# A reordered three-layer kernel: input splits moved to GpSimd, transposes and a layer norm spread between matmuls, and a new memory map

## The chip, the cores and the metric

The kernel runs on one core of one Trainium2 chip. The metric is the device time of one execution in microseconds (us). TensorE (PE) multiplies, VectorE (DVE), ScalarE (ACT) and GpSimd (POOL) work on tiles, and SyncE (SP) issues the loads. DVE and ACT read the accumulation banks that PE fills; POOL works on tiles in the on-chip memory only. Pairs below are numbered q0 to q27 over the whole kernel.

## The reference

Three layers, cut to what matters here (b = 2 batches, 768 positions, 512 features, all float32):

```python
x  = window_and_block_attention(q, k, v)             # (2, 768, 512)
h  = relu(x.transpose(0, 2, 1) @ w_tok1) @ w_tok2    # mixing over positions
u  = x + h.transpose(0, 2, 1)
u  = u + relu(u @ w_ch1) @ w_ch2                     # 1536 hidden columns
xn = (u - mean(u)) / sqrt(var(u) + 1e-6) * g_ln
out = u + relu(xn @ w2_ch1) @ w2_ch2                 # 2048 hidden columns
```

## The kernel before, in words

Each float32 matmul is made of three matmuls of rounded parts: every operand is split into a high part (a cast, on ACT) and a low part (the value minus the high part, one subtraction with both inputs in on-chip memory). The functions with names `high_...` and `low_...` make these parts.

**The up products.** The two channel layers are four groups, g = 0 to 3: layer and batch (0 and 1 are layer one on batch 0 and 1; 2 and 3 are layer two). A group has 6, 6, 8 and 8 pairs of 128-column hidden blocks (`PAIRS_OF`). For one pair, `up(q, i)` multiplies seven combinations of weight blocks and input blocks (a two by two Strassen scheme), i = 0 to 6, six matmuls of 384 columns each. The seven inputs of a group, `in_t[:, i]`, are three raw blocks of the transposed input (`raw_in`) and four sums of them, `t_in`, which POOL makes in `sum_inputs`; `high_input` and `low_input` split each. The products land alternately in two banks (`up_bank`). ACT copies product 0 to `p1`; DVE adds the others to `u2`, `u3` and three `c_raw` tiles. ACT and DVE turn four blocks into `hidden` (relu, high and low).

**The down products.** While PE works at the ups of pair q, it does between them the twelve units `down(q-1, t, f)` of the pair before, three matmuls of 512 columns each, into six banks that hold the group's output. `DOWNS_AFTER` says how many follow each up. `low_down` (DVE) and `high_down` (ACT) split the down weights, `low_up`, `high_up`, `high_sums`, `low_sums` the up weights of the next pair. `sum_weights` and `low_sums` are POOL's, for every pair.

**The next group's input.** It is transposed on PE in eight batches of three 128x128 transposes (`turn_batch`), copied by ACT (`copy_batch`). `BATCHES_AT[g][j]` says how many stand at the end of pair j of group g. They use the same two banks as the ups. Before the groups of layer two the input is normalised: `norm_before` (DVE, six statistics, then the moments and the variance) stands at the end of the second pair of the next group, ACT takes a square root, and `norm_after` (DVE, `to_turn`) stands at the end of the third.

**Group ends.** In the first pair of a group, DVE adds the finished output tiles of the group before (`add_out`). The inputs 0 to 3 of the next group are split in the last pair of a group, 4 to 6 in its first (`LATE_IN`), all low parts on DVE.

**Before q0.** After the attention, PE multiplies the second batch's mixing (`mix_hidden`, 12 groups of three matmuls; `mix_out`, six tiles of six matmuls), with batches 0 to 7 of group 0's input between, and q0 follows.

Every engine runs its own list in order; semaphores join them. A wait on one engine holds all that stands behind it there. Two memory maps lie over each other: the tiles of the attention and the mixing, and the tiles of the channel layers. A tile of the second map may be written only when what lies under it in the first is no longer read.

Of the kernel before, what the change touches and what calls it, by code (L numbers as in the profile page):

```python
# [44 lines left out]
PAD = 640  # L45
# [37 lines left out]
def build(nc, q_t, k_w, v_w, v_edge, v_t, w_tok1, w_tok2, w_ch1, w_ch2, w2_ch1, w2_ch2, gain, mask,  # L83
          value_init, identity, out):
    ctx = ExitStack()
    with ctx:
# [19 lines left out]
        with ExitStack() as a:  # L106
# [15 lines left out]
            tok_stage = sb(a, "tok_stage", [P, S])  # L122
            tok_w = sb(a, "tok_w", [P, 2, TOK_CH, S], F32R)
            x_split = sb(a, "x_split", [P, B, 2, NT, DM], F32R)
# [78 lines left out]
        in_low = sem("in_low")  # L203
        up_done = sem("up_done")
# [56 lines left out]
        def _(sp):  # L261
# [99 lines left out]
        def _(pool):  # L361
# [62 lines left out]
            def sum_inputs(g):  # L424
                def blk(j, k):
                    return raw_in[:, 2 * j:2 * j + 2, k * HN:(k + 1) * HN]

                if g:
                    pool.wait_ge(in_low, 7 * g)
                tt = nc.gpsimd.tensor_tensor  # L430
# [5 lines left out]
                pool.wait_ge(t_made, 4 * g + 2)  # L436
                tt(t_in[:, 2], blk(1, 1), blk(0, 1), ALU.subtract).then_inc(t_made, 1)
                pool.wait_ge(t_made, 4 * g + 3)
                pool.wait_ge(in_copied, 8 * g + 8)
# [25 lines left out]
            sum_inputs(0)  # L465
            for q in range(1, NQ):
                g, j = group_of(q)
                if q + 1 < NQ:
                    sum_weights(q + 1)
                    low_sums(q + 1)  # L470
                if g + 1 < NGROUP and j == T_AT[g]:
                    sum_inputs(g + 1)


        @block.tensor
        def _(pe):
# [135 lines left out]
            for t in range(GT):  # L612
                mix_hidden(1, 1, t, score_bank[0])
            pe.wait_ge(x_low_end, 2)
# [3 lines left out]
            first_batch(2)  # L618
            first_batch(3)
            for t in range(NT):  # L620
                if t == 0:
                    pe.wait_ge(x_done, 2 * NPAIR)
                    pe.wait_ge(h_low, 4)
                if t >= 2:
                    pe.wait_ge(u_done, NT + t - 1)
                for m in range(2):
                    mix_out(t, m, o_bank[t % 2])
                if t < 4:
                    first_batch(4 + t)

            def up(q, i):
# [4 lines left out]
                if j == 0:  # L636
                    pe.wait_ge(in_low, 7 * g + i + 1)
# [23 lines left out]

            def pair(q):
# [3 lines left out]
                units = iter(UNITS)  # L666
                for i in range(7):
# [22 lines left out]
                    up(q, i)  # L690
                    if q:
                        for _ in range(DOWNS_AFTER[i]):
                            down(q - 1, *next(units))
                for b in range(BATCHES_AT[g][j]):
                    if g and turned % 8 == 0 and b == 0:
                        pe.wait_ge(nat_ready, NT * g)
# [4 lines left out]
                    turn_batch(turned + b)  # L701

# [7 lines left out]
        def _(act):  # L710
# [41 lines left out]
            def copy_batch(k):  # L752
# [3 lines left out]
                if g and i == 0:  # L756
                    act.wait_ge(in_low, 7 * g)
                    act.wait_ge(t_made, 4 * g)
# [39 lines left out]
            def pair(q):  # L798
# [12 lines left out]
                high_hidden(q, 0, product_bank(q, 2)[:, 0:HN])  # L811
                if q and q + 1 < NQ:
# [14 lines left out]
                if g in (1, 2) and j == 1:  # L827
                    act.wait_ge(ln_step, LN_STEPS * g)
                    nc.scalar.activation(dev[:], var[:], ACT.Sqrt).then_inc(dev_done, 1)
# [34 lines left out]
            copy_batch(1)  # L864
            for m in range(2):
                high_h(1, m, score_bank[1 - m])
                copy_batch(2 + m)
            high_input(0, 0)
            for k in range(4, 8):
                copy_batch(k)  # L870
            for i in range(1, 7):
# [6 lines left out]
        def _(dve):  # L878
# [85 lines left out]
            def norm_before(ln):  # L964

                dve.wait_ge(mixed, NT * (ln + 1))
                for j in range(NT):
                    nc.vector.bn_stats(stats[:, j, :], natural[:, NT * ln + j, :]).then_inc(ln_step, 1)
# [7 lines left out]
            def norm_after(ln):  # L976
# [15 lines left out]
                for j in range(NT):  # L992
                    nc.vector.tensor_scalar(to_turn[:, j, :], natural[:, NT * ln + j, :],  # L993
# [173 lines left out]
```

## Time and profile before

| | |
|---|---|
| median of 3 runs | 664.21 us (663.83 to 666.57) |
| profiled execution, its own time | 664.86 us |
| its span | 663.1 us |
| mean granted TensorE clock | 0.964 of full speed |
| PE busy | 598.0 us, 90% |
| DVE busy | 359.4 us, 54% |
| POOL busy | 247.2 us, 37% |
| ACT busy | 244.9 us, 37% |

The span lies within the execution's own time and is 1.76 us shorter. A busy figure is the sum of an engine's instructions; PE's is overstated a little, since the ends of its matmuls are modelled.

### The profile page before, as it was taken

Reading aid. Unit: us, or ns where it says so; the run is one execution under the profiler, and the core shown is the slowest. Engines: PE = TensorE matmul, PEld = TensorE weight load, DVE = VectorE, ACT = ScalarE, POOL = GpSimd, SP = SyncE. Lnnn points to the kernel's source line nnn. Section 1 sums busy time; section 2 is a strip of 40 time slices with the busy share of each in tenths; the row PEclk is TensorE's granted clock in tenths of the full one; section 3 lists DMA queues with packets and bytes.
Section 4 is the critical chain, followed back from the end, with each engine's and each line's share of the span. In section 5 each row is a group of like instructions: output and inputs, shape, how many; then the busy total and the mean of one; then the engine's idle time right before and its main releaser. Section 6 shows DMA issues by size and latency. Waiting matters only on the chain.

```text
span 663.1 us, 8253 instructions
## 1 busy us (share of the span) xinstructions
PE 598.0 (90%) x2976; PEld 513.7 (77%) x2976; DVE 359.4 (54%) x695; ACT 244.9 (37%) x450; POOL 247.2 (37%) x247
## 2 busy tenths in 40 slices
PE   5999998878999899986998798699998999999997
PEld 2777887757888787875787687588887788898896
DVE  5568656283444558654442876523445784444435
ACT  3577655242332235332323532233332633333321
POOL 5464744170333663320334533332227433333300
PEclk9899999898999989988999799889998999999999
DMA  8887540001111011111101111101111111111302
GB/s 230 238 232 217 162 130 2 1 0 64 63 65 63 2 63 64 64 63 64 63 20 46 64 63 64 63 1 64 64 64 63 65 63 65 64 64 63 128 0 96
DMA packets 24896, 50.34 MB, mean 76 GB/s; under 512 B 7596, under 2 KB 7832, under 8 KB 24856
## 3 DMA queue, kind: packets, MB, share of 16 engines
q1 hardware_dynamic: 24304, 49.37, 22.6%
q10 hardware_dynamic: 552, 0.44, 0.3%
q8 instruction: 24, 0.39, 0.2%
q14 instruction: 16, 0.13, 0.1%
HBM read 46.07 MB, written 3.15 MB: 74 GB/s over the span
## 4 chain that ended last, share of the span: by engine, by line
PE 65%; DVE 18%; ACT 8%; issue 5%; POOL 1%; DMA 1%; SPq 0%; DVEq 0%; ACTq 0%; POOLq 0%
PE bank L478 63%; DVE down_w L880 5%; DVE hidden L955 3%; ACT hidden L796 3%; DVE in_t L880 3%; ACT down_w L792 2%; DVE c_raw L1022 2%; DVE c_raw L1028 1%; PE bank L571 1%; DVE c_raw L1036 1%; DVE neg_scores L898 1%; DVE to_turn L993 1%; DMA k_sb<-k_w 1%; ACT probs L723 1%; PE bank L513 1%
## 5 line engine op out<-in xcount | busy, mean ns | idle before, releaser
L478 PE MATMUL bank<-down_w,hidden 128*128 128x512 f32 x1008 | 272.2, 403 | 3.4 <-DVE hidden L955 3.3
L478 PEld LDWEIGHTS bank<-down_w,hidden 128*128 128x128 f32 x1008 | 191.5, 193 | 34.5 <-issue 5.4
L478 PE MATMUL bank<-in_t,up_odd 128*128 128x384 f32 x588 | 124.5, 348 | 10.4 <-DVE c_raw L1022 4.3
L478 PE MATMUL bank<-in_t,up_even 128*128 128x384 f32 x588 | 122.1, 345 | 12.4 <-ACT p L802 5.5
L478 PEld LDWEIGHTS bank<-in_t,up_odd 128*128 128x128 f32 x588 | 108.8, 195 | 22.5 <-issue 9.6
L478 PEld LDWEIGHTS bank<-in_t,up_even 128*128 128x128 f32 x588 | 107.8, 194 | 23.1 <-ACT p L802 6.7
L796 ACT ACTIVATE hidden<-c_raw 128x384 fp32r<-128x384 f32 x84 | 44.2, 527 | 216.6 <-DVE c_raw L1022 118.2
L420 POOL TENSOR_TENSOR up_even<-sums_up,up_even 128x1024 fp32r<-128x1024 f32 x14 | 33.5, 2396 | 158.8 <-ACT up_even L786 158.7
L420 POOL TENSOR_TENSOR up_odd<-sums_up,up_odd 128x1024 fp32r<-128x1024 f32 x14 | 33.6, 2400 | 145.5 <-ACT up_odd L786 145.5
L955 DVE SCALAR_TENSOR_TENSOR hidden<-c_raw,hidden 128x384 fp32r<-128x384 f32 x84 | 59.0, 702 | 48.0 <-ACT hidden L796 48.0
L1003 DVE TENSOR_TENSOR u<-bank,p 128x384 f32<-128x384 f32 x28 | 15.6, 557 | 69.5 <-PE bank L478 68.0
L880 DVE TENSOR_TENSOR down_w<-raw_down,down_w 128x1024 fp32r<-128x1024 f32 x28 | 46.0, 1642 | 3.2 <-ACT down_w L792 2.6
L796 ACT ACTIVATE hidden<-bank 128x384 fp32r<-128x384 f32 x28 | 13.8, 492 | 86.0 <-PE bank L478 86.0
L478 PE MATMUL bank<-k_sb,q_sb 128*128 128x364 f32 x96 | 39.1, 493 | 5.7 <-POOL k_sb L369 3.1
L723 ACT ACTIVATE probs<-neg_scores,neg_max 128x182 f32<-128x182 f32 x96 | 37.8, 443 | 13.9 <-DVE neg_max L898 13.3
L898 DVE CUSTOM_DVE_ANT_0 neg_scores<-bank,mask_sb 128x182 f32<-128x182 f32 x96 | 29.3, 343 | 22.8 <-PE bank L478 20.9
L1022 DVE TENSOR_TENSOR c_raw<-bank,u 128x384 f32<-128x384 f32 x28 | 15.6, 556 | 42.1 <-PE bank L478 42.1
L1014 DVE TENSOR_TENSOR u<-bank,p 128x384 f32<-128x384 f32 x28 | 15.6, 557 | 37.2 <-PE bank L478 37.2
L955 DVE SCALAR_TENSOR_TENSOR hidden<-bank,hidden 128x384 fp32r<-128x384 f32 x28 | 15.6, 557 | 35.4 <-ACT hidden L796 35.4
L732 ACT COPY probs_t<-bank 128x384 f32<-128x384 f32 x48 | 22.8, 474 | 30.3 <-PE bank L513 30.1
L792 ACT CAST down_w<-raw_down 128x1024 fp32r<-128x1024 f32 x28 | 29.0, 1037 | 0.0
L478 PE MATMUL bank<-v_own,probs_t 128*128 128x65 f32 x192 | 27.5, 267 | 0.0
(87 smaller groups left out, 724.2 us busy)
## 6 DMA issues: line engine op xcount, KB each, us to landing
raw_up<-w_ch SPq DMA_DIRECT2D x28, 512.0 KB, 4.3
raw_down<-w_ch SPq DMA_DIRECT2D x28, 512.0 KB, 3.5
k_sb<-k_w SPq DMA_DIRECT2D x16, 273.0 KB, 4.3
v_own<-v_w SPq DMA_DIRECT2D x8, 390.0 KB, 3.3
q_sb<-q_t SPq DMA_DIRECT2D x8, 384.0 KB, 5.4
v_turned<-v_t SPq DMA_DIRECT2D x8, 384.0 KB, 3.4
out<-natural SPq DMA_DIRECT2D x12, 256.0 KB, 3.1
tok_stage<-w_tok SPq DMA_DIRECT2D x4, 384.0 KB, 3.9
```

Of the source, the lines that this page charges most:

```text
L420: nc.gpsimd.tensor_tensor(w[:, 1, 3:7, :], sums_up[:], w[:, 0, 3:7, :].bitcast(F32), ALU.subtract).then_inc(sums_low, 1)
L478: return nc.tensor.matmul(dst, lhs, rhs, start=start, stop=stop, skip_group_check=True)
L723: nc.scalar.activation(probs[:, n % 2, h * NK:(h + 1) * NK], neg_scores[:, n % 2, h, :], ACT.Exp, bias=neg_max[:, n % 2, h:h + 1], scale=- ...
L732: nc.scalar.copy(probs_t[:, n % 2, :], turn_bank[n % 2][:, 0:3 * P]).then_inc(turned_copied, 1)
L792: nc.scalar.copy(down_w[:, q % 2, :, 0, :], raw_down[:, q % 2]).then_inc(down_high, 1)
L796: nc.scalar.activation(hidden[:, q % 2, f, 0, h * HN:(h + 1) * HN], src, ACT.Relu).then_inc(hid_high, 1)
L880: return nc.vector.tensor_tensor(dst, src, high.bitcast(F32), ALU.subtract)
L898: nc.vector.tensor_tensor_reduce(neg_scores[:, n % 2, h, :], score_bank[n % 3][:, h * NK:(h + 1) * NK], mask_sb[:, kind, (1 - h) * NSUM:(1 ...
L955: nc.vector.scalar_tensor_tensor(out=hidden[:, q % 2, f, 1, at], in0=src, scalar=0.0, in1=hidden[:, q % 2, f, 0, at].bitcast(F32), op0=ALU ...
L1003: nc.vector.tensor_tensor(u2[:], product_bank(q, 1)[:, 0:HN], p1[:], ALU.add).then_inc(u_made, 1)
L1014: nc.vector.tensor_tensor(u3[:], product_bank(q, 3)[:, 0:HN], p1[:], ALU.add).then_inc(u_made, 1)
L1022: nc.vector.tensor_tensor(c_raw[:, 0], product_bank(q, 4)[:, 0:HN], u3[:], ALU.add).then_inc(c_made, 1)
```

## The change

The matmuls are the same in number and shape, and no load is added or left out. What changes is who does some steps, and where they stand:

- Of each group's seven low inputs DVE keeps 0 and 1 (`DVE_IN = 2`); POOL makes 2 to 6. They count on a semaphore of their own. In group 0, POOL makes 2 to 4 between its `t_in` sums.
- The six `mix_out` tiles of batch 1 stand after the ups 0 to 5 of q0. q0 has no transposes any more; group 0's pairs q1 to q4 have two batches each, group 1's q8 to q10 have 3, 3, 2.
- In pairs with batches the downs are spread: one or two stand behind each batch too.
- `norm_before` and `norm_after` are cut into pieces between the steps of the first two pairs of a group. The square root stands earlier on ACT.
- The second `c_raw` sum stands ahead of `low_down` on DVE.
- `sum_inputs` comes one pair earlier in groups 1 and 2.
- The memory map: `down_w` lies behind `raw_in`, under what the attention used; `hidden` lies higher, over parts of the second batch's x and the mixing weights; `x_split` and `tok_w` have changed places; `pad` is gone. The first two loads of `raw_down` wait for all four `mix_hidden` results (`tok1_done` 4) in place of the first two.

The core of the diff:

```diff
-DOWNS_AFTER = (2, 2, 2, 2, 1, 1, 2)
+DOWNS_AFTER = {0: (2, 2, 2, 2, 1, 1, 2), 2: (2, 2, 1, 1, 1, 1, 1, 1, 2), 3: (2, 1, 1, 1, 1, 1, 1, 1, 1, 2)}
-BATCHES_AT = ((2, 2, 2, 2, 0, 0), (0, 0, 2, 3, 3, 0), (0, 0, 2, 2, 2, 2, 0, 0), (0,) * 8)
-T_AT = (4, 5, 6)
+BATCHES_AT = ((0, 2, 2, 2, 2, 0), (0, 0, 3, 3, 2, 0), (0, 0, 2, 2, 2, 2, 0, 0), (0,) * 8)
+T_AT = (4, 4, 5)
+DVE_IN = 2
...
             raw_in = sb(b_, "raw_in", [P, C, S])
+            down_w = sb(b_, "down_w", [P, 2, 2, 2, DM], F32R)
+            in_t = sb(b_, "in_t", [P, 7, 2, 2, HN], F32R)
             t_in = sb(b_, "t_in", [P, 4, 2, HN])
-            in_t = sb(b_, "in_t", [P, 7, 2, 2, HN], F32R)
+            up_odd = sb(b_, "up_odd", [P, 2, 7, 2 * P], F32R)
+            raw_down = sb(b_, "raw_down", [P, 2, 2, DM])
             p1 = sb(b_, "p1", [P, HN])
             u2 = sb(b_, "u2", [P, HN])
             u3 = sb(b_, "u3", [P, HN])
+            c_raw = sb(b_, "c_raw", [P, 3, HN])
             hidden = sb(b_, "hidden", [P, 2, 2, 2, S], F32R)
-            pad = sb(b_, "pad", [P, PAD])
-            up_odd = sb(b_, "up_odd", [P, 2, 7, 2 * P], F32R)
-            raw_down = sb(b_, "raw_down", [P, 2, 2, DM])
-            down_w = sb(b_, "down_w", [P, 2, 2, 2, DM], F32R)
             to_turn = sb(b_, "to_turn", [P, NT, DM])
-            c_raw = sb(b_, "c_raw", [P, 3, HN])
...
                 else:
-                    sp.wait_ge(tok1_done, 2)
+                    sp.wait_ge(tok1_done, 4)
                 sp.dma_start(raw_down[:, q % 2], down_v[g // 2][j]).then_inc(ld_down[q % 2], 16)
...
+            def low_input(g, i):
+                pool.wait_ge(in_high, 7 * g + i + 1)
+                src = t_in[:, T_OF[i]] if i in T_OF else raw_block(i)
+                nc.gpsimd.tensor_tensor(in_t[:, i, 1], src, in_t[:, i, 0].bitcast(F32), ALU.subtract
+                                        ).then_inc(in_low_pool, 1)
+                pool.wait_ge(in_low_pool, (7 - DVE_IN) * g + i - DVE_IN + 1)
...
             sum_inputs(0)
+            low_input(0, 5)
+            low_input(0, 6)
             for q in range(1, NQ):
                 g, j = group_of(q)
+                if j == 0:
+                    for i in range(LATE_IN, 7):
+                        low_input(g, i)
                 if q + 1 < NQ:
                     sum_weights(q + 1)
                     low_sums(q + 1)
                 if g + 1 < NGROUP and j == T_AT[g]:
                     sum_inputs(g + 1)
+                if g + 1 < NGROUP and j == PAIRS_OF[g] - 1:
+                    for i in range(DVE_IN, LATE_IN):
+                        low_input(g + 1, i)
...
                     up(q, i)
+                    if q == 0 and i < NT:
+                        last_mix(i)
                     if q:
-                        for _ in range(DOWNS_AFTER[i]):
+                        for _ in range(after[i]):
                             down(q - 1, *next(units))
...
                     turn_batch(turned + b)
+                    for _ in range(after[7 + b]):
+                        down(q - 1, *next(units))
```

On ACT, the order ahead of q0 becomes copies 0 to 3, `high_input(0, 0)`, copy 4, `high_h(1, 0)`, copy 5, `high_input(0, 1)`, copy 6, `high_h(1, 1)`, copy 7, `high_input(0, 2)` to `(0, 6)`, and then the pairs. On DVE, a pair becomes, with the pieces for a group's second pair (`scaling`) shown:

```diff
                 nc.vector.tensor_tensor(u2[:], product_bank(q, 1)[:, 0:HN], p1[:], ALU.add).then_inc(u_made, 1)
-                if opening:
-                    for i in range(LATE_IN, 7):
-                        low_input(g, i)
+                if scaling:
+                    row_stats(g - 1, 4)
+                    row_stats(g - 1, 5)
...
+                if scaling:
+                    row_moments(g - 1)
                 dve.wait_ge(up_done, 7 * q + 4)
...
                 low_hidden(q, 1, c_raw[:, 0])
-                low_down(q)
...
                 dve.wait_ge(up_done, 7 * q + 6)
                 nc.vector.tensor_tensor(c_raw[:, 1], product_bank(q, 5)[:, 0:HN], u3[:], ALU.add).then_inc(c_made, 1)
-                if ending:
-                    low_input(g + 1, 2)
-                    low_input(g + 1, 3)
+                low_down(q)
                 low_hidden(q, 2, c_raw[:, 1])
...
-                if g in (1, 2) and j == 1:
-                    norm_before(g - 1)
-                if g in (1, 2) and j == 2:
-                    norm_after(g - 1)
```

`row_stats(ln, 0)` to `(ln, 3)` stand behind the `add_out` of the group's first pair, `row_scales` behind `u3` of the second, and two `normed` tiles behind each of its last three hidden blocks.

## Rows read from the trace of the kernel before

**Rows 1.** The page, busy time of the engine (share of the span) and instructions.

```profile
PE 598.0 (90%) x2976; PEld 513.7 (77%) x2976; DVE 359.4 (54%) x695; ACT 244.9 (37%) x450; POOL 247.2 (37%) x247
```

**Rows 2.** Windows: length, busy time by engine, granted clock (PEclk), DMA share, GB/s.

```profile
core 0: us, PE busy (x) PEld busy (x) DVE busy (x) ACT busy (x) POOL busy (x), PEclk, DMA share, GB/s
158.49:213.92 55.43, 51.92 (x253) 45.55 (x253) 23.10 (x34) 17.75 (x31) 16.68 (x15) 0.97 0.16 57
213.92:283.46 69.54, 65.61 (x312) 57.37 (x313) 43.00 (x55) 25.11 (x39) 31.94 (x24) 0.98 0.14 51
283.46:331.23 47.77, 38.79 (x173) 33.22 (x171) 24.07 (x49) 14.41 (x24) 10.90 (x10) 0.89 0.18 64
331.23:405.64 74.41, 67.89 (x321) 59.44 (x322) 41.72 (x54) 27.20 (x42) 32.76 (x24) 0.95 0.12 44
405.64:451.66 46.02, 36.99 (x169) 32.07 (x168) 24.07 (x49) 12.79 (x23) 10.89 (x10) 0.89 0.16 62
451.66:523.95 72.29, 67.23 (x325) 58.51 (x325) 35.30 (x44) 24.73 (x40) 31.95 (x24) 0.98 0.13 49
523.95:557.00 33.05, 31.96 (x156) 28.09 (x157) 22.54 (x34) 12.77 (x20) 12.16 (x10) 1.00 0.19 66
557.00:635.36 78.36, 78.36 (x392) 70.48 (x390) 37.83 (x56) 25.30 (x40) 24.63 (x21) 1.00 0.22 80
231.76:250.40 18.64, 17.74 (x79) 15.24 (x79) 11.34 (x14) 7.96 (x13) 11.06 (x10) 0.91 0.16 56
```

**Rows 3.** Timeline of q8, the layer norm: start, us, engine, line, [idle before <-releaser].

```profile
285.66 3.65 DVE L968 BATCH_NORM_STATS2 stats<-natural 128x6 f32<-128x512 f32 x6
...
290.59 1.60 PE L478 MATMUL bank<-in_t,up_even 128*128 128x384 f32 x6 [2.10 <-ACT p L802]
...
308.76 1.54 PE L571 MATMUL bank<-ident,to_turn 128*128 128x128 f32 x6 [5.56 <-DVE to_turn L993]
```

**Rows 4.** Timeline of PE: an up and two downs; the batches at the end of q1.

```profile
256.54 1.21 PE L478 MATMUL bank<-in_t,up_even 128*128 128x384 f32 x6
...
257.59 1.55 PE L478 MATMUL bank<-down_w,hidden 128*128 128x512 f32 x6
...
176.92 0.55 PE L571 MATMUL bank<-ident,natural 128*128 128x128 f32 x3 [0.69 <-DVE c_raw L1036]
...
177.94 1.28 PE L478 MATMUL bank<-in_t,up_even 128*128 128x384 f32 x6 [0.47 <-ACT raw_in L761]
```

**Rows 5.** Timeline of q4, where POOL makes the sums of the next input.

```profile
226.10 1.85 POOL L435 TENSOR_TENSOR t_in<-raw_in,t_in 128x768 f32<-128x768 f32 x1
226.13 2.24 DVE L955 SCALAR_TENSOR_TENSOR hidden<-c_raw,hidden 128x384 fp32r<-128x384 f32 x1 [0.59 <-ACT hidden L796]
...
228.03 2.04 POOL L437 TENSOR_TENSOR t_in<-raw_in 128x768 f32<-128x768 f32 x1
...
228.29 2.86 DVE L880 TENSOR_TENSOR down_w<-raw_down,down_w 128x1024 fp32r<-128x1024 f32 x1
...
231.76 1.29 PE L478 MATMUL bank<-in_t,up_odd 128*128 128x384 f32 x6 [1.95 <-DVE c_raw L1028]
```

**Rows 6.** Timeline of DVE, the same two operations with POOL idle.

```profile
300.46 1.23 DVE L880 TENSOR_TENSOR down_w<-raw_down,down_w 128x1024 fp32r<-128x1024 f32 x1 [0.39 <-ACT down_w L792]
...
304.37 0.56 DVE L955 SCALAR_TENSOR_TENSOR hidden<-c_raw,hidden 128x384 fp32r<-128x384 f32 x1 [0.59 <-ACT hidden L796]
```

**Rows 7.** Groups by line on POOL: count, busy us, mean ns of one, idle before.

```profile
L440 POOL TENSOR_TENSOR t_in<-raw_in,t_in 128x768 f32<-128x768 f32 x4 | 10.2, 2561 | 0.3
...
L435 POOL TENSOR_TENSOR t_in<-raw_in,t_in 128x768 f32<-128x768 f32 x4 | 7.4, 1843 | 3.1 <-ACT raw_in L761 2.8
```

**Rows 8.** Timeline ahead of q0 and in it.

```profile
121.22 6.37 PE L478 MATMUL bank<-x_split,tok_w 128*128 128x512 f32 x27
...
129.18 0.86 ACT L774 CAST in_t<-raw_in 128x768 fp32r<-128x768 f32 x1
...
142.55 0.47 ACT L802 COPY p<-bank 128x384 f32<-128x384 f32 x1
```

**Rows 9.** The page's loads: count, KB each, us from issue to landing.

```profile
raw_down<-w_ch SPq DMA_DIRECT2D x28, 512.0 KB, 3.5
```

More of the change, by code:

```diff
@@ L44 @@
 KB = 3
-PAD = 640
 AHEAD = 3
@@ L617, in _ @@
                     mix_hidden(1, m, t, score_bank[1 - m])
[L618 to L629, printed above, removed]
+                first_batch(4 + 2 * m)
+                first_batch(5 + 2 * m)
             def up(q, i):
@@ L635, in up @@
                 use[0] += 1
-                if j == 0:
-                    pe.wait_ge(in_low, 7 * g + i + 1)
+                if j == 0 and i < DVE_IN:
+                    pe.wait_ge(in_low, DVE_IN * g + i + 1)
+                if j == 0 and i >= DVE_IN:
+                    pe.wait_ge(in_low_pool, (7 - DVE_IN) * g + i - DVE_IN + 1)
                 for c in range(2):
@@ L660, in down, with last_mix @@
                     last.then_inc(down_done, 1)
+            def last_mix(t):
+                if t == 0:
+                    pe.wait_ge(x_done, 2 * NPAIR)
+                    pe.wait_ge(h_low, 4)
+                if t >= 2:
+                    pe.wait_ge(u_done, NT + t - 1)
+                for m in range(2):
+                    mix_out(t, m, o_bank[t % 2])
             def pair(q):
@@ L666, in pair @@
                 units = iter(UNITS)
+                after = DOWNS_AFTER[BATCHES_AT[g][j]]
                 for i in range(7):
@@ L690, in pair @@
                     up(q, i)
+                    if q == 0 and i < NT:
+                        last_mix(i)
                     if q:
-                        for _ in range(DOWNS_AFTER[i]):
+                        for _ in range(after[i]):
                             down(q - 1, *next(units))
                 for b in range(BATCHES_AT[g][j]):
-                    if g and turned % 8 == 0 and b == 0:
-                        pe.wait_ge(nat_ready, NT * g)
+                    if turned % 8 == 0 and b == 0:
+                        if g:
+                            pe.wait_ge(nat_ready, NT * g)
+                        else:
+                            pe.wait_ge(u_done, 2 * NT)
                     if b < 2:
@@ L811, in pair @@
                 high_hidden(q, 0, product_bank(q, 2)[:, 0:HN])
+                if g in (1, 2) and j == 1:
+                    act.wait_ge(ln_step, LN_STEPS * g)
+                    nc.scalar.activation(dev[:], var[:], ACT.Sqrt).then_inc(dev_done, 1)
                 if q and q + 1 < NQ:
@@ L863, in _ @@
             high_x(2 * NPAIR - 1)
-            copy_batch(1)
+            for k in range(1, 4):
+                copy_batch(k)
+            high_input(0, 0)
             for m in range(2):
+                copy_batch(4 + 2 * m)
                 high_h(1, m, score_bank[1 - m])
[L867 to L871, printed above, removed]
+                copy_batch(5 + 2 * m)
+                if m == 0:
+                    high_input(0, 1)
+            for i in range(2, 7):
                 high_input(0, i)
@@ L962, in add_out, with row_stats, row_moments @@
                 nc.vector.tensor_tensor(tile, acc_bank[t][:], tile, ALU.add).then_inc(mixed, 1)
[L964 to L968, printed above, removed]
+            def row_stats(ln, j):
+                dve.wait_ge(mixed, NT * ln + j + 1)
+                nc.vector.bn_stats(stats[:, j, :], natural[:, NT * ln + j, :]).then_inc(ln_step, 1)
+            def row_moments(ln):
                 for j in range(NT):
@@ L991, in norm_after, with normed @@
                     dve.wait_ge(in_turned, 8 * (ln + 2))
-                for j in range(NT):
-                    nc.vector.tensor_scalar(to_turn[:, j, :], natural[:, NT * ln + j, :],
-                                            moments[:, j, 0:1], r[:, 3, j:j + 1],
-                                            ALU.subtract, ALU.mult).then_inc(nat_ready, 1)
+            def normed(ln, j):
+                nc.vector.tensor_scalar(to_turn[:, j, :], natural[:, NT * ln + j, :],
+                                        moments[:, j, 0:1], rstd[:, 3, j:j + 1],
+                                        ALU.subtract, ALU.mult).then_inc(nat_ready, 1)
             def pair(q):
@@ L1000, in pair @@
                 opening = g > 0 and j == 0
+                normed_group = g in (1, 2)
+                scaling = normed_group and j == 1
+                if q == 0:
+                    add_mixed(1, 0, o_bank[0])
                 dve.wait_ge(up_done, 7 * q + 2)
@@ L1039, in pair @@
                     add_out(g - 1, 5)
-                if g in (1, 2) and j == 1:
-                    norm_before(g - 1)
-                if g in (1, 2) and j == 2:
-                    norm_after(g - 1)
+                    if normed_group:
+                        row_stats(g - 1, 3)
+                if scaling:
+                    normed(g - 1, 4)
+                    normed(g - 1, 5)
             nc.vector.memset(warm[:], 0.0).then_inc(warm_ready, 1)
@@ L1087, in _ @@
                 low_h(1, m, score_bank[1 - m])
-            for t in range(NT):
-                add_mixed(1, t, o_bank[t % 2])
-                if t >= 2:
-                    low_input(0, t - 2)
-            for i in range(4, 7):
+            for i in range(DVE_IN):
                 low_input(0, i)
```

49 lines of the change are left out of this document (40 added, 9 removed).

## The prediction

> **What bounds the kernel now.** I read the page first: PE is busy for 90% of the span [rows 1], so time can come only from what keeps PE waiting or slows it, and no work of PE's goes away. Then I cut the span at the first up matmul of each pair and read windows [rows 2]. The last row but one is the measure of all: from 557.00 to 635.36 PE is busy all the time at the full clock (2.4 GHz), five pairs in 78.36 us, 15.67 us a pair. By that, q1 to q21 would take 329 us and their 22 batches (0.5 us each on PE [rows 4]) 11 us, 340 in all. The first seven windows of [rows 2] sum to 398.5 us. So some 58 us are lost between 158.49 and 557.00, and this is what the change goes for. The largest parts are the two windows of 47.77 and 46.02 us, which hold the layer norms. The timeline there [rows 3] shows DVE in six statistics when ACT's `p` copy and the next ups need it (PE idle 2.10 us), and then PE idle 5.56 us for the normalised tiles; the granted clock of the window is 0.89, for after such gaps PE runs at 1.2 GHz for a while.
>
> **Prices.** An up is 1.05 us (257.59 less 256.54 [rows 4]), a down (15.67 - 7 x 1.05)/12 = 0.69. A batch adds 0.5. Now the first of two batches has no down behind it, and PE waits 0.69 and 0.47 us [rows 4]. With one or two downs behind each batch those waits are covered: DVE's sum takes about 0.55 and a copy 0.47 [rows 8] against a down of 0.69. I take 16.9 us for a pair with two batches (15.67 + 1.0, and 0.25 for what doesn't fit) and 17.3 with three. A stretch at half clock costs half its length: in the window of 231.76 to 250.40 the clock is 0.91, so (1 - 0.91) x 18.64 = 1.7 us. I charge 1.7 for every PE gap over 2 us.
>
> **POOL and DVE.** The trace has no low input on POOL. The nearest rows are its sums of the same shape, also with two inputs in on-chip memory: 1.84 us on average at one line, 2.56 at another that overlaps more of DVE's work [rows 7]. I take 1.85, the row without other work. Twenty of them are 37 us of POOL, which is idle half its time; what matters is what they do to DVE. In q4 the `hidden` low part began 0.03 us after a POOL sum and took 2.24 us, and `low_down` began during the next sum and took 2.86 [rows 5]; with POOL idle they take 0.56 and 1.23 [rows 6]. Both DVE operations have two inputs in on-chip memory. So each costs up to 1.7 more when it meets a POOL sum, and PE waited 1.95 us for the `c_raw` sum behind them [rows 5].
>
> The Trainium skill (SBUF — State Buffer, section "Who interferes with whom") says that a DVE instruction with two SBUF inputs and a GpSimd instruction that reads SBUF exclude each other for the whole instruction. Rows 5 agree in kind, but not fully: `low_down` ended 1.08 us after the sum at 228.03 ended, sooner than its 1.23. Taken strictly the rule speaks against the move and would add about 0.8 us to each of five places below, 4 us in all.
>
> **Part by part, against before.** Pair ends are counted from the same cuts.
>
> *Ahead of q0 and q0: +0.9.* The 27 mixing matmuls take 0.23 each [rows 8]; with three pairs of batches between them PE is through at about 130.4. ACT has `high_input(0, 1)` between copies 5 and 6, and it waits for `t_in[1]`: copy 5 at 128.7, POOL 1.85, a cast of 0.84, so copies 6 and 7 end at 133.0. After a cast, POOL goes on with low 2, a sum, low 3, low 4 and the last sum: five of 1.85, one cast of ACT between, gaps of 0.1, from 133.9 to 144.8. ACT's casts 5 and 6 follow, and only then the `p` copy of q0, as now: 146.9, where it is 142.55 to 143.0 before [rows 8]. Up 2 waits for it; what stood before q0 (mixing tiles 0 and 1) and ups 0 and 1 lie ahead and are covered. From there 5 ups and 4 mixing tiles of 1.38 are 10.8 us, plus 1.7 for the clock: q1 starts at 159.4 instead of 158.49. Bounds: -3 if POOL meets no DVE work and the clock holds, +5 at 2.56 us a step. The delayed load hides: released at 129.5 and 3.5 us a load [rows 9], three loads land by 140, and `high_down` of q0 wants the first after 150.
>
> *q1 to q3: -4.7.* 3 x 16.9 = 50.7, before 55.43. What is saved is the clock after q0's end and the batch waits.
>
> *q4 to q7: +3.7.* Before 69.54. q4 has two batches now and POOL's sums as before. Spreading the downs brings the last `c_raw` sum, needed by the second batch, 2.1 us nearer to the ups. I follow DVE: low hidden 1 until a sum ends, `c_raw`, `low_down` until the next one ends, low hidden 2 behind a third, then `c_raw`: PE waits 3.0 us (bounds 2.0, as rows 5, and 3.8, all blocked in full). 15.67 + 1.0 for the batches + 3.0 = 19.7. q5: 15.67 + 1.7 for the clock = 17.4. In its end POOL makes low 2 and 3 while DVE has `low_down` and low hidden 2, so the first down of q6 comes 1.8 late. In q6 POOL makes low 4 to 6 before `sum_weights(7)`, four pieces before the next `high_sums`; ACT stands in that, and behind it the relu and DVE's chain with four statistics more. q6: 15.67 + 1.8 + 0.6 = 18.1; q7: 15.67 + 2.0 + 0.3 = 18.0. Together 73.2. Bounds 65 (no collision shows on PE) to 79.
>
> *q8 and q9: -13.2.* 2 x 17.3 = 34.6 against 47.77. The statistics lie in the gaps of q6 and q7 (where DVE has only a pair's own work it is busy 37.83 us in five pairs, 7.6 each [rows 2], so 8 us of a pair are free; the six statistics take 3.65 [rows 3], and the normalised tiles lie in the next pair). If that cover were gone, up to the 2.10 and 5.56 would come back.
>
> *q10 to q13: -1.2.* As q4 to q7, with two batches in q10: 73.2 against 74.41. Before, ACT waited in q11 for `t_in[1]`; that goes, and q10 pays the collision.
>
> *q14, q15: -12.2.* 2 x 16.9 against 46.02.
>
> *q16 to q19: -2.5.* 16.9 + 19.7 + 17.4 + 15.8 = 69.8 against 72.29.
>
> *q20, q21: +1.3.* 18.1 + 16.3 = 34.4 against 33.05: q20 takes the collision of q19's end.
>
> *From q22 on: 0.* Nothing of the change is there but `c_raw` ahead of `low_down`, and PE is already never idle.
>
> *Memory map: 0.* 1008 down matmuls read `down_w` and `hidden` at new places. Now matmuls of 512 columns run at 0.23 us on the mixing tiles [rows 8] and on the down weights (0.69/3 [rows 2, 4]), at quite different places, so I see no price of place.
>
> The sum: 0.9 - 4.7 + 3.7 - 13.2 - 1.2 - 12.2 - 2.5 + 1.3 = -27.9. The profiled execution took 664.86, so 637.0; it stands 0.65 above the median of the runs, so **636.3**.
>
> **Rivals.**
> 1. *The forecast*, collisions of POOL and DVE eat half of what the order could give: 627 to 646. Chance 0.55.
> 2. *The collisions mostly miss PE.* The three waits of 3.0 and three of 1.8 and their clock charges (3 x 1.7), and 4 of the ACT waits in the openings, go: about 17 to 20 us more, 616 to 627. For it: DVE is under 60% busy and PE has two banks; against it: rows 5. Chance 0.21.
> 3. *Each collision costs a whole POOL operation and a clock dip behind it*, in the group ends, the openings and q0: about 4 us more at four places, 646 to 658. For it: rows 5 and the charge of the skill's rule. Chance 0.16.
> 4. *Slower than before.* POOL's list becomes the chain of the group ends: it makes 20 low inputs and 16 sums, 36 x 1.85 = 67 us. If PE stood behind most of them it would lose the 27.9 and more; from 15 of the 36 on (28 us) with PE idle beside what I counted it decides: 665 to 680. Against it: in q5 and q11 ups 2 and 3 want their low inputs 4 us after I have them made. Chance 0.04.
> 5. *The map matters, or the reordering only shifts the waits*: the tiles for q8 come late and both norm gaps return at the new place, 2 x (2.1 + 5.6 + 1.7) = 19 us back, 652 to 660. Against it: the statistics start a whole pair earlier. Chance 0.04.
>
> **Numbers.** The likeliest is case 1, 636.3, with its own range 627 to 646. The range to hold the time 8 times in 10 takes 0.55 of case 1, about 0.15 of case 2 and 0.10 of case 3: 619 to 653. A run of this kernel can tell about 0.5% (3.3 us) from no change. Faster 0.95, same 0.01, slower 0.04.
>
> **What would show it.** In the profile after: no wait of PE for `to_turn` over 1 us; q8, q9, q14, q15 near 17 us each at full clock; waits of PE near 3 us for the last `c_raw` at the end of q4, q10 and q17; `hidden` low parts and `low_down` over 2 us beside POOL's low inputs; a wait of PE at up 2 of q0 for `p`, ending near 147; five pairs from q22 still 15.67 each. I am wrong if the low inputs on POOL take far more than 2.5 us, if the down matmuls' rate is no longer 0.23, or if ACT's early waits for POOL in q0 and the openings hold more than 2 us.

## The result and the profile after

The changed kernel takes 645.89 us (median of 4 runs, 642.85 to 647.12) against 664.27 before: ratio 0.971, 95% interval 0.9668 to 0.9751. The forecast was 636.3, range 619 to 653. Its profiled execution took 647.12, 17.7 us less than the one of before, where the sum of the prediction said 27.9.

The first view is that of windows, cut where q0, q1, q4, q8, q10, q14, q16, q20 and q22 of the changed kernel begin, and after five more pairs. Columns as in [rows 2].

```profile
136.90:162.95 26.05, 20.05 (x78) 17.53 (x79) 10.67 (x15) 6.00 (x9) 15.95 (x11) 0.80 0.05 19
162.95:212.24 49.29, 49.29 (x254) 43.89 (x254) 23.92 (x36) 18.14 (x31) 19.86 (x15) 1.00 0.22 80
212.24:288.11 75.87, 68.87 (x320) 59.81 (x318) 50.35 (x69) 26.86 (x42) 42.04 (x29) 0.93 0.13 46
288.11:322.26 34.15, 33.84 (x174) 29.63 (x175) 19.15 (x30) 14.19 (x24) 13.24 (x10) 1.00 0.25 93
322.26:399.98 77.72, 70.19 (x319) 61.02 (x318) 50.30 (x69) 25.76 (x41) 41.99 (x29) 0.91 0.12 41
399.98:433.47 33.49, 33.17 (x169) 29.19 (x170) 19.15 (x30) 13.04 (x22) 13.24 (x10) 1.00 0.24 87
433.47:502.41 68.94, 65.96 (x326) 58.83 (x324) 33.72 (x44) 24.82 (x39) 30.07 (x21) 0.98 0.14 50
502.41:539.74 37.33, 33.63 (x158) 29.27 (x157) 24.27 (x30) 12.30 (x19) 24.34 (x19) 0.95 0.15 57
539.74:618.09 78.35, 78.35 (x391) 70.51 (x390) 35.59 (x55) 26.07 (x41) 24.64 (x21) 1.00 0.22 81
```

Against [rows 2], pair by pair group:

| | before | forecast | after |
|---|---|---|---|
| q1 to q3 | 55.43 | 50.7 | 49.29 |
| q4 to q7 | 69.54 | 73.2 | 75.87 |
| q8, q9 | 47.77 | 34.6 | 34.15 |
| q10 to q13 | 74.41 | 73.2 | 77.72 |
| q14, q15 | 46.02 | 33.8 | 33.49 |
| q16 to q19 | 72.29 | 69.8 | 68.94 |
| q20, q21 | 33.05 | 34.4 | 37.33 |

The rest is q1's start, 162.95 against 158.49 (+4.5, forecast +0.9), and -0.5 from q22 to the end. Of the 4.5, 2.6 lie ahead of the second batch's first mixing matmul (118.81 against 116.25). In the profiles of the other kernels below, all with the same attention code, that point lies anywhere from 115.7 to 120.3, and on one chip from 116.53 (`p_first`) to 120.30 (`pool_order`). So these 2.6 us are within what it varies by from one profiled execution to another, and I don't count them as the change's.

The whole list of PE's waits shows what is left. Columns: who waited for whom, us in total, times, longest. The view is that of waits from 116 us on.

```profile
PE bank L591 <- DVE c_raw L1097: 9.1, 3, 3.0
PE bank L498 <- DVE c_raw L1084: 8.3, 5, 2.7
PE bank L498 <- ACT p L832: 6.0, 1, 6.0
PE bank L498 <- DVE in_t L912: 3.8, 1, 3.8
PE bank L498 <- DVE x_split L912: 3.0, 1, 3.0
PE bank L498 <- issue: 2.2, 3, 1.1
PE bank L498 <- DVE hidden L987: 2.2, 5, 0.5
```

No wait for `to_turn` is left, where [rows 3] had 5.56 us. The three waits of 3.0 us stand at the last batch of q4, q10 and q17. The timeline of q4's end shows how they come about, as in [rows 5]:

```profile
224.31 2.04 POOL L435 TENSOR_TENSOR t_in<-raw_in,t_in 128x768 f32<-128x768 f32 x1
...
225.05 2.40 DVE L912 TENSOR_TENSOR down_w<-raw_down,down_w 128x1024 fp32r<-128x1024 f32 x1
...
226.44 2.67 POOL L439 TENSOR_TENSOR t_in<-raw_in 128x768 f32<-128x768 f32 x1
227.37 2.15 DVE L987 SCALAR_TENSOR_TENSOR hidden<-c_raw,hidden 128x384 fp32r<-128x384 f32 x1
...
230.04 0.90 PE L591 MATMUL bank<-ident,natural 128*128 128x128 f32 x3 [3.04 <-DVE c_raw L1097]
```

DVE's two operations take 2.40 and 2.15 against 1.23 and 0.56 [rows 6], and the `c_raw` sum stands behind both. The 6.0 us are q0's, and there POOL and ACT are the chain:

```profile
145.75 1.80 POOL L445 TENSOR_TENSOR t_in<-raw_in,t_in 128x768 f32<-128x768 f32 x1
...
147.58 0.83 ACT L804 CAST in_t<-t_in 128x768 fp32r<-128x768 f32 x1 [5.03 <-POOL t_in L445]
...
149.05 0.47 ACT L832 COPY p<-bank 128x384 f32<-128x384 f32 x1
...
149.57 2.29 PE L498 MATMUL bank<-in_t,up_even 128*128 128x384 f32 x6 [6.00 <-ACT p L832]
```

Of the 8.3 us, 7.5 stand right before the first up of a group's second pair (2.67 before q7, 2.70 before q13, 2.10 before q21), so they are in the windows of q6, q12 and q20. They are larger than forecast. The timeline of q6 has their cause. ACT waits 6.09 us for the last of POOL's `sum_weights`, which stand behind low inputs 4 to 6; the relu comes late, so the low hidden part falls into POOL's `low_sums` and takes 2.49; and the second `c_raw` sum ends so late that PE stands 2.67 us before q7:

```profile
261.78 0.73 POOL L414 TENSOR_TENSOR sums_up<-raw_up,sums_up 128x256 f32<-128x256 f32 x1
...
262.55 1.05 ACT L816 CAST up_odd<-sums_up 128x1024 fp32r<-128x1024 f32 x1 [6.09 <-POOL sums_up L414]
...
263.74 2.40 POOL L420 TENSOR_TENSOR up_odd<-sums_up,up_odd 128x1024 fp32r<-128x1024 f32 x1 [1.22 <-ACT up_odd L816]
...
264.06 2.49 DVE L987 SCALAR_TENSOR_TENSOR hidden<-c_raw,hidden 128x384 fp32r<-128x384 f32 x1 [2.64 <-ACT hidden L826]
...
268.35 2.26 PE L498 MATMUL bank<-in_t,up_odd 128*128 128x384 f32 x6 [2.67 <-DVE c_raw L1084]
```

### The profile page after: what moved, and what is told of

The parts are those of the page before. It is cut to its first block, busy times and chain, and to the rows that moved or that the text cites. A ratio compares the mean times of both kernels' runs of the same rounds, so it can differ in the third digit from the quotient of the medians.

```text
span 645.3 us, 8274 instructions
## 1 busy us (share of the span) xinstructions
PE 595.6 (92%) x2976; PEld 514.4 (80%) x2976; DVE 356.1 (55%) x675; ACT 244.6 (38%) x450; POOL 290.6 (45%) x267
## 4 chain that ended last, share of the span: by engine, by line
PE 71%; DVE 12%; POOL 6%; issue 4%; ACT 4%; DMA 2%; SPq 1%; POOLq 0%; ACTq 0%; DVEq 0%
PE bank L498 68%; DVE hidden L987 4%; POOL in_t L451 3%; DVE down_w L912 2%; PE bank L591 2%; DMA tok_stage<-w_tok 1%; ACT hidden L826 1%; ACT in_t L804 1%; DMA k_sb<-k_w 1%; DVE c_raw L1084 1%; DVE c_raw L1070 1%; DVE neg_scores L930 1%; ACT probs L753 1%; PE bank L533 1%; PE bank L531 1%
## 5 line engine op out<-in xcount | busy, mean ns | idle before, releaser
L498 PE MATMUL bank<-down_w,hidden 128*128 128x512 f32 x1008 | 278.0, 405 | 4.5 <-issue 2.2
L498 PEld LDWEIGHTS bank<-down_w,hidden 128*128 128x128 f32 x1008 | 189.5, 193 | 33.7 <-issue 5.9
L498 PEld LDWEIGHTS bank<-in_t,up_odd 128*128 128x128 f32 x588 | 109.5, 195 | 18.4 <-issue 8.7
L987 DVE SCALAR_TENSOR_TENSOR hidden<-c_raw,hidden 128x384 fp32r<-128x384 f32 x84 | 75.9, 904 | 39.4 <-ACT hidden L826 39.4
L912 DVE TENSOR_TENSOR down_w<-raw_down,down_w 128x1024 fp32r<-128x1024 f32 x28 | 39.5, 1412 | 0.0
L412 POOL TENSOR_TENSOR sums_up<-raw_up 128x256 f32<-128x256 f32 x28 | 28.4, 1014 | 2.2
```

The source lines that it names most:

```text
L412: tt(sums_up[:, S3], raw[:, A11], raw[:, A21], ALU.subtract).then_inc(up_sum, 1)
L498: return nc.tensor.matmul(dst, lhs, rhs, start=start, stop=stop, skip_group_check=True)
L912: return nc.vector.tensor_tensor(dst, src, high.bitcast(F32), ALU.subtract)
L987: nc.vector.scalar_tensor_tensor(out=hidden[:, q % 2, f, 1, at], in0=src, scalar=0.0, in1=hidden[:, q % 2, f, 0, at].bitcast(F32), op0=ALU ...
```

## Experiments

Times are medians; a ratio is to the kernel before on the same chip, with its 95% interval. Differences between two kernels of this section, or to the changed kernel's 645.9, are between medians. All compute the whole reference.

### One step of POOL: `pool_order`

```diff
                 if q + 1 < NQ:
-                    sum_weights(q + 1)
+                    if j or q == 1:
+                        sum_weights(q + 1)
                     low_sums(q + 1)
...
                 if g + 1 < NGROUP and j == PAIRS_OF[g] - 1:
+                    sum_weights(q + 2)
                     for i in range(DVE_IN, LATE_IN):
                         low_input(g + 1, i)
```

> The changed kernel with one POOL step moved: in a group's last pair, sum_weights for the second pair ahead stands before low inputs 2 and 3, so that in the group's first pair only low 4 to 6 and low_sums are left. Theory (ACT's high_sums waits for POOL's list, and the relu and DVE's chain behind it come late): q6, q7, q12, q13, q20, q21, now 18.6 to 20.4 us each, fall to 16 to 16.8, together 15 to 20 us less, 626 to 631 us. Rival (the first pairs are late because DVE has output tiles and statistics to do while POOL's instructions block it, whatever the order): 0 to 4 us less, 642 to 646.

628.48 us, ratio 0.9448 (0.9417 to 0.9478): 17.4 less, as the theory said. q6, q7, q12, q13, q20 and q21 are now 17.07, 17.21, 17.12, 17.18, 17.07 and 15.90, 101.6 us where they were 116.0, so 14.4 us of it lie there. The waits before q7, q13 and q21 are gone. In q6, q12 and q20 PE waits 1.2 us for a `hidden` low part, which is why the pairs stay above the 16 to 16.8 of the theory. The queue order on POOL alone cost 17 us.

### POOL's sums at another place: `sums_early`

```diff
                 if q + 1 < NQ:
                     sum_weights(q + 1)
+                    if g + 1 < NGROUP and j == T_AT[g]:
+                        sum_inputs(g + 1)
+                    if g + 1 < NGROUP and j == T_AT[g] + 1:
+                        last_sum(g + 1)
                     low_sums(q + 1)
-                if g + 1 < NGROUP and j == T_AT[g]:
-                    sum_inputs(g + 1)
```

(For groups 1 to 3 `sum_inputs` now makes the first three sums and waits for six batches before the first of them; `last_sum` makes the fourth.)

> The changed kernel with POOL's first three t_in sums of groups 1 to 3 between sum_weights and low_sums of the same pair, where DVE has little with two inputs in memory, and the fourth at that place of the next pair. Theory (three waits of PE of 3.0 us, each with a stretch at half clock, come from DVE's low hidden and low_down being blocked by these sums): q4, q10, q17 fall from 21.1, 21.1, 20.0 to about 16.6 with two batches, together 12 to 14 us less, 632 to 634. Rival (the sums block low_up and the last low hidden at the new place, and the wait moves to the ups 3 and 4): 0 to 5 us less, 641 to 646.

631.08 us, ratio 0.9491 (0.9465 to 0.9517): 14.8 less. q4, q10, q17 are 16.40, 16.43 and 16.72, and their waits are gone. The same sums cost PE nothing where DVE has little with two inputs in memory: in q4 `low_up` took 2.00 us beside the third sum, 0.95 without one, and no wait of PE followed.

### ACT's order in q0: `p_first`

```diff
-            for i in range(2, 7):
+            for i in range(2, 5):
                 high_input(0, i)
...
                 high_hidden(q, 0, product_bank(q, 2)[:, 0:HN])
+                if q == 0:
+                    high_input(0, 5)
+                    high_input(0, 6)
```

> The changed kernel with ACT's casts of inputs 5 and 6 of group 0 behind the first relu of q0, so that the p copy no longer waits for POOL's last t_in sum. Theory (PE's 6.0 us before up 2 of q0 come from ACT's order alone): p is copied near 143, PE waits under 1 us there, q1 starts 6 to 9 us earlier, 637 to 640. Rival (POOL's list of nine steps holds q0, so PE waits at up 5 or 6 for its low inputs instead): 0 to 3 us less, 643 to 646.

636.61 us, ratio 0.9571 (0.9545 to 0.9598): 9.3 less. q0 takes 17.32 us where it took 26.05, which is 8.7: 6.0 of wait, and 2.7 of PE's busy time (20.05 to 17.32), which is the clock.

### The memory map alone: `map_only`

The kernel before with the new map and the wait for `tok1_done` 4; the lines are those of the diff above.

> The kernel before with nothing but the new memory map and the wait of the first raw_down loads for tok1_done 4. Theory (place costs nothing): 664.3 within 1.5 us; 36 down matmuls in a row in 8.3 us as before; the attention's end is where it was. Rival (the map or the later loads are a part of the result, or cost the 2.6 us by which the attention ended later in the profile of the changed kernel): outside 662 to 667, with the difference before 120 us or in the rate of the down matmuls.

665.05 us, ratio 0.9995 (0.9979 to 1.0012). Five pairs from q22 take 78.4 us as before. The map and the later first loads cost and give nothing.

### The norm in blocks, the rest new: `norm_blocks`

Statistics, moments, variance and square root at the end of a group's second pair, scales and tiles at the end of the third, as before the change.

> The changed kernel with the layer norm put back in its two blocks (statistics, moments and square root at the end of a group's second pair, scales and tiles at the end of the third), all else new. Theory (the norm's spread is worth what q8, q9, q14, q15 lost: 47.77 + 46.02 before against 34.15 + 33.49 after, less what the statistics cost in the first pairs): 18 to 26 us more than the changed kernel, 664 to 672. Rival (these pairs gained by the spread downs, the norm itself mattered little): under 8 us more, under 654.

657.63 us, ratio 0.9879 (0.9834 to 0.9924): 11.7 more, between the theory and the rival. q8 is 27.38 instead of 17.36 and q14 25.89 instead of 17.05, 18.9 together; but q6, q7, q12 and q13, freed of pieces of the norm, take 74.1 instead of 78.7. The spread pays 19 and, with POOL's queue as it was, gave 4.6 of it back in the pairs that took the work.

### The downs close together: `downs_close`

```diff
-DOWNS_AFTER = {0: (2, 2, 2, 2, 1, 1, 2), 2: (2, 2, 1, 1, 1, 1, 1, 1, 2), 3: (2, 1, 1, 1, 1, 1, 1, 1, 1, 2)}
+DOWNS_AFTER = {n: (2, 2, 2, 2, 1, 1, 2) + (0,) * n for n in (0, 2, 3)}
```

> The changed kernel with all twelve downs behind the seven ups again and the batches at the end of a pair with nothing between. Theory (11 pairs with batches, q1 to q4, q8 to q10 and q14 to q17, lose the covered waits of 1.2 to 1.6 us each, but the three pairs with POOL's sums lose less): 10 to 16 us more, 656 to 662. Rival (the downs moved behind the batches only shift waits to the later ups): 0 to 5 us more.

646.39 us, ratio 0.9725 (0.969 to 0.976): 0.5 more, no difference. The rival's size, but not its reason. q1 to q3 are 16.9 instead of 16.43, and q8, q9 18.04 and 17.48 instead of 17.36 and 16.79, so the spread is worth 0.5 to 0.7 a pair. q4, q10, q17 are 19.26, 19.37 and 19.36 instead of 21.06, 21.10 and 19.99: with the downs spread, the ups stand closer and the last `c_raw` sum is wanted sooner, so the waits for it are 3.0 us there and 2.0 here. And 16.9 was surprising. With two batches and nothing between them the kernel before needs 18.0. Something else had taken 1.1 us per pair.

### The low inputs back on DVE: `lows_dve`

For groups 1 to 3 only; low 4 to 6 stand behind `u2` of the first pair, 2 and 3 at the end of the last; `lows_before` counts them.

```diff
                 if opening:
+                    for i in range(LATE_IN, 7):
+                        low_input(g, i)
...
                 low_hidden(q, 3, c_raw[:, 2])
+                if ending:
+                    low_input(g + 1, 2)
+                    low_input(g + 1, 3)
```

> The changed kernel with the low inputs 2 to 6 of groups 1 to 3 on DVE again (2 and 3 at the end of the last pair of a group, 4 to 6 behind u2 in the first); group 0 stays on POOL. Theory (first pairs are late by POOL's list, not by DVE's amount): q6, q7, q12, q13, q20, q21 fall by 1 to 3 us each, 633 to 640. Rival (moving them to POOL was what paid, DVE is too full in first pairs with statistics): 646 to 655.

622.20 us, ratio 0.9361 (0.9335 to 0.9388): 23.7 less, more than the theory said and 6 more than by POOL's order alone. Windows of q6 and q7, first the changed kernel, then this one:

```profile
249.09:268.35 19.26, 16.06 (x79) 13.88 (x78) 14.34 (x17) 6.84 (x11) 16.59 (x13) 0.98 0.15 55
268.35:288.11 19.76, 19.00 (x79) 15.99 (x79) 16.90 (x32) 6.55 (x11) 7.54 (x7) 0.85 0.15 54
```

```profile
246.41:262.06 15.65, 15.65 (x79) 14.08 (x78) 14.46 (x23) 7.25 (x11) 5.63 (x5) 1.00 0.20 68
262.06:278.63 16.57, 16.02 (x80) 13.89 (x78) 14.80 (x32) 6.13 (x10) 5.62 (x5) 1.00 0.18 64
```

DVE, third busy figure, has 17 instructions in q6 of the changed kernel and 23 in this one, five of them the low inputs 2 to 6 of 0.95 us each, and is busy 14.34 and 14.46 us. The work taken from DVE came back to it as time blocked by POOL: in the changed kernel, between 248.48 and 268.35, `low_up` took 2.50 us where it takes 0.95, and three `hidden` low parts took 2.20, 1.06 and 2.49 where they take 0.56. But that is not the whole of the 23.7. `pool_order` left the low inputs on POOL and took 17.4, so most of the cost was where they stood in POOL's queue, and 6.3 is what they cost beyond it.

### Three edits together: `three`

`pool_order`, `sums_early` and `p_first` in one kernel.

> The three single edits together: sum_weights ahead of low 2 and 3, POOL's sums between sum_weights and low_sums, inputs 5 and 6 behind the first relu of q0. Theory (three separate waits): their gains add, 17.4 + 14.8 + 9.3 = 41.5 us, 604 us, within 3. Rival (they share idle time of POOL: the fourth sum of groups 1 and 2 now stands in the last pair, which also takes a second sum_weights): 608 to 615.

607.95 us, ratio 0.9149 (0.913 to 0.9167): 37.9 less than the changed kernel, of the 41.5 that the three add up to. 1.9 of the remaining 3.6 is q1, 18.31 us: low hidden 1 of q0 now falls beside POOL's low 6, and the first down waits 1.65 us for the mixing's last tile.

### One step of DVE on the kernel before: `craw_first`

```diff
                 low_hidden(q, 1, c_raw[:, 0])
-                low_down(q)
...
                 nc.vector.tensor_tensor(c_raw[:, 1], product_bank(q, 5)[:, 0:HN], u3[:], ALU.add).then_inc(c_made, 1)
+                low_down(q)
```

> The kernel before with one DVE step moved: low_down behind the second c_raw sum, not ahead of it. Theory after downs_close (in pairs with batches it is this order, not the spread downs, that took most of the waits at the batches: such pairs are 16.9 with the downs close together and 18.0 before): q1 to q3, q9, q10 and q15 to q17 fall by 1.0 to 1.3 us each, 8 to 11 us less, 653 to 657. Rival (the order helps only where the rest of the change is there): within 2 us of 664.

645.76 us, ratio 0.9724 (0.9693 to 0.9755): 18.5 less, and 8 more than expected. This one moved call, on the kernel before, gives what the whole change gives. The end of q2, first in the kernel before and then here:

```profile
191.14 1.64 DVE L880 TENSOR_TENSOR down_w<-raw_down,down_w 128x1024 fp32r<-128x1024 f32 x1
...
192.70 0.55 DVE L1028 TENSOR_TENSOR c_raw<-bank,u 128x384 f32<-128x384 f32 x1
...
193.84 0.56 DVE L955 SCALAR_TENSOR_TENSOR hidden<-c_raw,hidden 128x384 fp32r<-128x384 f32 x1 [0.59 <-ACT hidden L796]
...
194.31 0.55 DVE L1036 TENSOR_TENSOR c_raw<-bank,u 128x384 f32<-128x384 f32 x1
```

```profile
188.62 0.54 DVE L1027 TENSOR_TENSOR c_raw<-bank,u 128x384 f32<-128x384 f32 x1
...
189.09 1.29 DVE L880 TENSOR_TENSOR down_w<-raw_down,down_w 128x1024 fp32r<-128x1024 f32 x1
...
190.30 0.55 DVE L955 SCALAR_TENSOR_TENSOR hidden<-c_raw,hidden 128x384 fp32r<-128x384 f32 x1
...
190.77 0.55 DVE L1036 TENSOR_TENSOR c_raw<-bank,u 128x384 f32<-128x384 f32 x1
...
191.32 0.82 PE L571 MATMUL bank<-ident,natural 128*128 128x128 f32 x6
...
192.47 1.28 PE L478 MATMUL bank<-in_t,up_odd 128*128 128x384 f32 x6 [0.33 <-ACT raw_in L761]
```

After the second `c_raw` sum DVE must wait for ACT's relu of it. Before, it stood idle there for 0.59 us; here `low_down` fills that time. From the first `c_raw` sum of the pair to the last it takes 4.11 us (186.66 to 190.77) instead of 5.27 (189.04 to 194.31). So the last `c_raw` sum is ready when PE wants its second batch, and both batches run as six transposes in a row, where PE waited 0.69 to 0.72 between them [rows 4]. q1 to q3 take 50.76 us against 55.43, q8 and q9 42.40 against 47.77, q14 and q15 42.28 against 46.02.

The eight pairs that the theory named gain 10.1 us, as expected. What it left out is mostly q8 and q14, with 3.4 us each: in q8 the wait for `p` is 0.94 instead of 2.10, the one for `to_turn` 4.81 instead of 5.56, and PE's busy time is 1.5 less.

### The edits that go together: `best`, `best_close`, `best_q0`

`best` is `lows_dve`, `sums_early` and `p_first`. `best_close` has the downs close together as well.

> The changed kernel with low inputs 2 to 6 of groups 1 to 3 on DVE, POOL's sums between sum_weights and low_sums, and inputs 5 and 6 of group 0 behind the first relu. Theory (POOL's low inputs in the first pairs, POOL's sums beside low_down, and ACT's order in q0 are three separate costs): 622.2 less 13.5 less 9.3, 599 us, within 3, with first and second pairs of a group at 15.7 to 16.6. Rival (DVE becomes late where it has low inputs and no longer waits for sums): 603 to 608, no better than the three edits with POOL.

> The kernel of the run best with the downs close together again. Theory (without POOL's sums beside them the spread downs are worth what they are in q1 to q3, 0.46 us a pair): 4 to 6 us more than best. Rival (no worth at all, as in the changed kernel, 0.5 us): within 1 us of best.

`best` takes 601.70 us, ratio 0.9061 (0.903 to 0.9091), and `best_close` 607.23, ratio 0.9144 (0.9113 to 0.9175): 5.5 more. `best` is in the range of its theory, with q6, q12 and q20 at 15.65. With POOL out of the way the spread downs are worth 0.4 to 0.7 us in every pair with batches. `best` has these waits of PE left from 116 us to 640:

```profile
PE bank L502 <- DVE in_t L920: 3.8, 1, 3.8
PE bank L502 <- DVE x_split L920: 3.0, 1, 3.0
PE bank L502 <- DVE natural L974: 1.7, 1, 1.7
PE bank L502 <- DVE c_raw L1095: 1.1, 2, 0.5
PE bank L502 <- DVE hidden L995: 0.6, 2, 0.3
```

The first of them is what `best_q0` goes for, with one cast of ACT moved (against `best`):

```diff
                 copy_batch(5 + 2 * m)
-                if m == 0:
-                    high_input(0, 1)
-            for i in range(2, 5):
+            for i in range(1, 5):
                 high_input(0, i)
```

> The kernel of the run best with ACT's cast of input 1 of group 0 behind copies 6 and 7 and the last relu of the mixing. Theory (ACT's wait for POOL's second sum there delays DVE's low input 0, for which PE waits 3.8 us before up 0): 2 to 3.5 us less than best. Rival (POOL's lows then come later by the same): within 1 us of best.

599.34 us, ratio 0.9029 (0.9 to 0.9059): 2.4 less than `best`, and the fastest here, 46.5 less than the changed kernel.

## Why the prediction came out as it did

**The measured time lies in the range, 9.6 us above the forecast.** The direction and the pattern were right: gains where the norm and the batches were, losses in q4 to q7 and q20, q21, and the map at nothing, which `map_only` shows.

**The waits in q4, q10 and q17** were forecast at 3.0 us each by following DVE through POOL's sums, and are 3.04, 3.04 and 2.98. That they come from where the sums stand is shown by `sums_early`. The clock's charge fell in the same pair and not in the next (q4 21.06 and q5 15.79, forecast 19.7 and 17.4), with nearly the same sum there, 36.85 against 37.1; q10 and q11 took 38.08.

**q8, q9, q14 and q15**: 67.6 us, forecast 68.4. The windows are right. What they were put down to is half right: `norm_blocks` shows 19 us from the norm in q8 and q14, of the 26.1 that the four pairs gained. The moved `low_down` is the other part that a run shows: `craw_first` alone takes 9.1 us off these four pairs.

**Ahead of q0 and q0**: forecast +0.9, measured +1.9 without the part that comes from elsewhere. The wait for `p` was seen ahead, "ending near 147"; it ended at 149.57, which is 147.0 with the 2.6 us of the attention taken off; `p_first` shows that it was ACT's order, not POOL's amount.

**The term that was mis-sized is the first and second pairs of a group**: "q6: 15.67 + 1.8 + 0.6 = 18.1; q7: 15.67 + 2.0 + 0.3 = 18.0", the same for q12 and q13, and 18.1 and 16.3 for q20 and q21. That is 106.6 us for six pairs and they took 116.0. The miss of the whole is 10.2 us between profiled executions (17.7 less instead of 27.9); 9.4 of it are these pairs, and the other terms miss by 3.6 for q1's start, by 1.0 in q10 and q11, and by nearly as much the other way elsewhere. The mechanism named there was the right one (low 4 to 6 before `sum_weights`, ACT's `high_sums` behind it), but its parts were mis-sized. The first down of q6, forecast 1.8 us late, waited 0.53. The late relu, for which I charged 0.6 us in q6 and 2.0 in q7, cost more: the low hidden part behind it fell beside `low_sums` and took 2.49 us where it takes 0.56. Without that the wait of 2.67 would have been about 0.7 (an estimate, 2.67 less 1.93). And that gap was followed by a stretch at half clock in q7 (granted clock 0.85, some 3 us of 19.76). I had left out the clock charge there, since my gaps came out under 2 us. `pool_order` takes 14.4 us off these six pairs, and `lows_dve` 20.2.

**A reason that fell.** For q1 to q3 the prediction said that "with one or two downs behind each batch those waits are covered". The waits went, but `downs_close` shows them going without the spread, and `craw_first` shows what took them: `low_down` behind the second `c_raw` sum. The prediction named this step only for the pairs from q22 on and gave it no price; there indeed it has none. The spread downs take 0.5 us a pair on top, and lose 3.3 again in the pairs where POOL's sums stand (q4 and q5, q10 and q11, q17 and q18 of the changed kernel against `downs_close`).

**What the change is made of.** `craw_first` alone is worth 18.5 us and the norm's spread 19 gross, 14 net of what it costs the pairs that took the work. The spread downs are worth 0.5 in the changed kernel, which is no difference, and 5.5 in `best`. On the other side, POOL's low inputs cost 24 in groups 1 to 3, 17 of it by their place in the queue, and ACT's order in q0 9. The place of the `t_in` sums costs 15, but the kernel before paid for its own place of them too: there PE waited 1.95 us before q5, 4.33 in q11 and 1.94 before q19. q4 and q5, q10 and q11, and q17 to q19 took 36.48, 41.04 and 54.18 us before and 36.85, 38.08 and 52.54 after. So this is a cost that the change left standing more than one that it brought. These parts overlap and are not to be added, but large gains and large losses stood in one change and left 18.4. No run takes the batches out of q0 or moves `sum_inputs` by itself, so what these two are worth is not shown.

**The rivals.** The time lies in case 1's own range (627 to 646), at the edge of case 3 (646 to 658, collisions worse in four places). Case 3's mechanism was there in the openings only. What the Trainium skill says (SBUF — State Buffer, section "Who interferes with whom"), that a VectorE instruction with two SBUF inputs and a GpSimd instruction that reads SBUF exclude each other, the traces bear out more closely than I had read it: the section on the hardware below has the numbers. The extra charge that I made of it, 0.8 us at each of five places, did not show in q4, q10 and q17, where the waits were those of the forecast.

## What to carry to other kernels

- Work that goes from VectorE to GpSimd is not gone from VectorE when both have two inputs in on-chip memory: five low inputs of 0.95 us left DVE's list in q6 and its busy time stayed at 14.4 us. Put it where VectorE is idle or reads one of its inputs from an accumulation bank.
- In a queue served in order, put first what another engine waits for next, and the filling work behind it. One moved call on DVE gave 18.5 us, one on POOL 17.4, two on ACT 9.3; no instruction was saved by any of them.
- When several parts change at once, price each step in each place where it stands, and take them apart afterwards. The net of 18 us hid more than 45 us that the same steps gave in a better order, with one of the moves taken back.

## What the runs showed of the hardware beyond that

- DVE and POOL take turns where both have two inputs in on-chip memory. A DVE operation that meets a running POOL one ends a fixed time after it, in the profiles of the kernel before, the changed one, `p_first` and `craw_first`: `low_down` 1.08 to 1.10 us after the end of a `t_in` sum (1.23 alone), a `hidden` low part 0.40 to 0.43 after that of a sum, a low input or `low_sums` (0.56 alone). Both are 0.13 to 0.16 us short of the time that the operation takes alone, so it waited for nearly all of the other's operation and then did its own. The POOL operation that starts meanwhile is stretched in the same way: 2.67 for a `t_in` sum and 2.94 for a low input, 1.82 to 1.85 alone.
- Size does not help the one that waits. In q7 a product of 128x6 numbers on DVE, both inputs in memory, took 2.39 us beside a `low_sums` of 2.40. In `lows_dve` a `TENSOR_SCALAR` of 128x6 with one input in memory took 2.27 and ended with the `low_sums` beside it; in the kernel before the same step took 0.17. But the 168 DVE operations of the changed kernel's pairs that read one of their inputs from a bank never took over 0.56 us, whatever POOL did.
- The 1.2 GHz stretch comes right behind the wait. After 2.67 us of wait before q7 six down matmuls took 2.90, which take 1.55 at the full clock; the granted clock was 0.62 from 268.35 to 276.43 and 1.00 from there to 288.11. In q4, where the wait lies inside the pair, so does the stretch (2.91 for six downs), and q5 is free of it (0.99).
